# Attention and two gated layers on one core: the order of evictions and weight parts in the second step of a block, and a shorter start

## What is computed

```python
scores = 0.125 * q @ k.T                      # 2 batches x 8 heads, 768 positions, 64 wide
keep   = (key < n_global) | (0 <= query - key < n_local)      # 8 and 96
scores = where(keep, scores - slope[head] * dist, -1e9)
a      = exp(scores - max); a = a / (sum(a) + 1e-9)
x      = (a @ v) laid out as 1536 tokens x 512
h = x @ w_in;   g = h * sigmoid(h);           x = g @ w_out     # 512 -> 2048 -> 512
h = x @ w_in2;  g = h * clip(h + 3, 0, 6) / 6;  y = g @ w_out2
```

## Time and profile before

| what | value |
|---|---|
| runs | 586.82, 587.07, 587.07 us; median 587.07 |
| the profiled execution: its own time | 586.97 us |
| its span, first to last instruction | 585.2 us |
| PE busy | 580.0 us (99%) |
| DVE busy, ACT busy, POOL busy | 361.9, 335.5, 266.7 us |
| chain of work that ended last | PE 97% |

### The profile page before, as it was taken

How to read it: one execution, slowest core, us unless ns; L and a number is a source line. 1 busy time by engine, 2 the same in 40 slices (tenths; PEclk the granted TensorE clock), 3 DMA queues, 4 the chain that set the end, 5 groups by cost and what they waited for, 6 DMA issues and landing times.

```text
span 585.2 us, 9670 instructions
## 1 busy us (share of the span) xinstructions
PE 580.0 (99%) x3476; PEld 522.5 (89%) x3476; DVE 361.9 (62%) x669; ACT 335.5 (57%) x652; POOL 266.7 (46%) x282
## 2 busy tenths in 40 slices
PE   9999999999999999999999999999999999999998
PEld 6788899999999999999999989999988988889996
DVE  7777887657545775586556685475448765555331
ACT  7998976554444774444447575445546754455441
POOL 6678774678333044394333343593330443331110
DMA  6665500422222122212221222222211262211002
GB/s 238 256 237 191 204 7 2 144 72 73 73 73 72 36 73 73 73 43 101 73 72 37 73 72 73 74 72 73 71 46 30 70 216 72 71 37 38 1 0 108
DMA packets 14883, 50.05 MB, mean 86 GB/s; under 512 B 1650, under 2 KB 2162, under 8 KB 14834
## 3 DMA queue, kind: packets, MB, share of 16 engines
q1 hardware_dynamic: 14402, 48.63, 24.5%
q10 hardware_dynamic: 432, 0.79, 0.4%
HBM read 46.27 MB, written 3.15 MB: 84 GB/s over the span
## 4 chain that ended last, share of the span: by engine, by line
PE 97%; DVE 1%; ACT 1%; issue 0%; DMA 0%; DVEq 0%
PE ps L1152 40%; PE ps L1243 23%; PE ps L1234 15%; PE ps L1235 8%; PE ps L1100 3%; PE ps L1124 3%; PE ps L1076 3%; PE ps L1109 1%; ACT probs L842 1%; DVE negs L623 0%; DMA words<-in_counts 0%; ACT probsT L853 0%; DVEq L232 0%; DVE m_base L568 0%; DVE x_raw L641 0%
## 5 line engine op out<-in xcount | busy, mean ns | idle before, releaser
L404 POOL TENSOR_TENSOR wo_lo<-wo_raw,wo_hi 128x1024 fp32r<-128x1024 f32 x32 | 77.3, 2415 | 260.1 <-ACT wo_hi L907 257.0
L1152 PE MATMUL ps<-x_hi,wi_hi 128*128 128x384 f32 x448 | 150.8, 337 | 0.1
L1152 PE MATMUL ps<-x_hi,wi_lo 128*128 128x384 f32 x448 | 150.0, 335 | 0.0
L1152 PE MATMUL ps<-x_lo,wi_hi 128*128 128x384 f32 x448 | 150.0, 335 | 0.0
L599 DVE TENSOR_TENSOR c_sb<-ps,p_c 128x384 f32<-128x384 f32 x64 | 35.6, 557 | 161.7 <-PE ps L1152 161.5
L887 ACT ACTIVATE p_c<-ps 128x384 f32<-128x384 f32 x64 | 31.5, 492 | 127.4 <-PE ps L1152 127.1
L1152 PEld LDWEIGHTS ps<-x_hi,wi_hi 128*128 128x128 f32 x448 | 84.1, 188 | 3.4 <-ACT u_c L887 0.9
L1152 PEld LDWEIGHTS ps<-x_hi,wi_lo 128*128 128x128 f32 x448 | 84.1, 188 | 0.7
L1152 PEld LDWEIGHTS ps<-x_lo,wi_hi 128*128 128x128 f32 x448 | 84.1, 188 | 0.0
L1243 PE MATMUL ps<-wo_hi,g_lo 128*128 128x512 f32 (+1 forms) x194 | 76.3, 393 | 0.0
L1243 PE MATMUL ps<-wo_lo,g_hi 128*128 128x512 f32 (+1 forms) x194 | 76.3, 393 | 0.0
(11 more groups left out here) (113 smaller groups left out, 1064.3 us busy)
## 6 DMA issues: line engine op xcount, KB each, us to landing
wi_raw<-in_w_in SPq DMA_DIRECT2D x32, 512.0 KB, 3.4
wo_raw<-in_w_out SPq DMA_DIRECT2D x32, 512.0 KB, 3.4
v_raw<-in_v SPq DMA_DIRECT2D x8, 704.0 KB, 4.0
k_raw<-in_kT SPq DMA_DIRECT2D x7, 464.0 KB, 5.1
out_y<-y_out SPq DMA_DIRECT2D x11, 256.0 KB, 4.1
q_raw<-in_qT SPq DMA_DIRECT2D x6, 384.0 KB, 6.0
q_raw<-in_qT ACTq DMA_DIRECT2D x1, 384.0 KB, 4.6
k_raw<-in_kT SPq DMA_DIRECT2D x1, 320.0 KB, 3.7
```

The source lines that it names most:

```text
L404: nc.gpsimd.tensor_tensor(wo_lo[:, s % 2, :], wo_raw[:, s % 2, :], wo_hi[:, s % 2, :], ALU.subtract).then_inc(wo_lo_ok, 1)
L1152: mm = nc.tensor.matmul(p_bank(bank), w[:, s % 2, at], x[:, b, k, :], start=fresh and k == 0 and i == 0, stop=k == 1 and i == 2, skip_grou ...
```

## The change

Three edits. In the steps called evict: on ACT `wo_high(s)` moves from before keep(P6) to behind y_copy(4); on DVE y_copy(3) comes from the end of the step before to behind c_sum(0), and w_low(s+1, 1) goes from behind c_sum(0) to behind c_sum(2). At the start: two of the three operations that lead to flag no longer depend on each other, `rows` becomes a zeroed 128x128 piece of y_out, the matmul that spreads the numbers has 128 columns in place of 5, one idle matmul fewer stands ahead of it, and POOL waits for `own_ok` before its two-input operation on the band tile (it waited for it later). In the attention: copy_t(2) goes from ACT to DVE, behind negations(2).

```diff
-        rows = sb("rows", [P, 9])
-        cnt = rows[0:1, :]
+        tests = sb("tests", [1, 2])
...
+        ones, rows = y_out[:, 0, 0:P], y_out[:, 1, 0:P]
+        cnt = y_out[0:1, 1, 0:P]
...
         def copied(u):
-            return (pt_dve, u // 2) if u % 2 and u > 1 else (pt_act, u + 1 if u < 2 else u // 2 + 2)
+            if u in (0, 1):
+                return pt_act, u + 1
+            if u == 2:
+                return pt_dve, 1
+            return (pt_dve, u // 2 + 1) if u % 2 else (pt_act, u // 2 + 1)
...
                 pool.wait_ge(far_ok, 1)
+                pool.wait_ge(own_ok, 1)
                 nc.gpsimd.tensor_tensor(m_base[:, BAND], rel8[:, BAND], far[:, BAND], ALU.subtract).then_inc(band_link, 1)
...
-                pool.wait_ge(own_ok, 1)
                 for r in range(NR):
...
-            nc.vector.memset(y_out[:, 0, 0:P], 1.0).then_inc(idle_ok, 1)
-            nc.vector.memset(rows[:, 4:9], 0.0).then_inc(chain, 1)
+            nc.vector.memset(ones, 1.0).then_inc(idle_ok, 1)
+            nc.vector.memset(rows, 0.0).then_inc(chain, 1)
...
+            nc.vector.tensor_scalar(tests[:, 0:1], cnt[:, 5:6], -1.0, MAXLOC + 1.0, ALU.mult, ALU.add).then_inc(chain, 1)
+            nc.vector.tensor_scalar(tests[:, 1:2], cnt[:, 4:5], float(GLOB), -NEVER, ALU.is_gt, ALU.mult).then_inc(chain, 1)
+            links[0] += 2
...
-            link(nc.vector.tensor_scalar(cnt[:, 0:1], cnt[:, 5:6], 1.0, None, ALU.is_ge))
-            link(nc.vector.scalar_tensor_tensor(cnt[:, 0:1], cnt[:, 5:6], float(MAXLOC), cnt[:, 0:1], ALU.is_le, ALU.mult))
-            nc.vector.scalar_tensor_tensor(flag[:, :], cnt[:, 4:5], float(GLOB), cnt[:, 0:1], ALU.is_le,
-                                           ALU.mult).then_inc(flag_ok, 1)
+            dve.wait_ge(chain, links[0])
+            nc.vector.scalar_tensor_tensor(flag[:, :], tests[:, 0:1], cnt[:, 5:6], tests[:, 1:2], ALU.mult,
+                                           ALU.is_gt).then_inc(flag_ok, 1)
...
-                nc.vector.tensor_copy(nums[:, :], ps[:, 1, 0:5]).then_inc(nums_ok, 1)
+                nc.vector.tensor_copy(nums[:, :], ps[:, 1, 4:9]).then_inc(nums_ok, 1)
...
                 negations(2)
+                copy_t(2)
                 negations(3)
...
                 if evict:
-                    w_low(s + 1, 1)
+                    y_copy(blk - 1, 3)
                     y_copy(blk - 1, 5)
                 c_sum(s, 1, 0, p5_c, P7)
                 c_sum(s, 2, 1, u2_c, P3)
+                if evict:
+                    w_low(s + 1, 1)
...
                     if blk > 0 and f == 0:
                         y_copy(blk - 1, 1)
-                        y_copy(blk - 1, 3)
...
                 exps(4)
-                copy_t(2)
                 exps(5)
...
                 if evict:
                     w_high(s + 1, 1)
                     y_copy(blk - 1, 2)
-                wo_high(s)
+                else:
+                    wo_high(s)
                 keep(s, u2_c, 0, P6)
                 keep(s, p5_c, 1, P5)
                 if evict:
                     y_copy(blk - 1, 4)
+                    wo_high(s)
...
-            busy(4)
+            busy(3)
             pe.wait_ge(row_ok, 3)
-            nc.tensor.matmul(ps[:, 1, 0:5], y_out[:, 0, 0:P], rows[:, 4:9], start=True, stop=True).then_inc(rows_ok, 1)
+            nc.tensor.matmul(ps[:, 1, 0:P], ones, rows, start=True, stop=True).then_inc(rows_ok, 1)
             busy(2)
```

More of the change, by code:

```diff
@@ L1057, in busy @@
                 for _ in range(n):
-                    nc.tensor.matmul(ps[:, 0, 0:P], y_out[:, 0, 0:P], y_out[:, 0, 0:P], start=True, stop=True)
-            busy(4)
+                    nc.tensor.matmul(ps[:, 0, 0:P], ones, ones, start=True, stop=True)
+            busy(3)
             pe.wait_ge(row_ok, 3)
-            nc.tensor.matmul(ps[:, 1, 0:5], y_out[:, 0, 0:P], rows[:, 4:9], start=True, stop=True).then_inc(rows_ok, 1)
+            nc.tensor.matmul(ps[:, 1, 0:P], ones, rows, start=True, stop=True).then_inc(rows_ok, 1)
             busy(2)
```

## The result

The changed kernel takes 581.84 us (median of 6 runs, 581.80 to 582.01) against 586.90 for the kernel before beside it (6 runs, 586.82 to 587.07): a ratio of 0.9913, 95% interval 0.9901 to 0.9926. The forecast was 585.4. The sign was right, but 5.06 us were gained and 1.66 forecast.

A forecast was written before the change was run, and what follows sets the result against it. PE, busy 99% of the span, bounds the kernel, so only its late starts can gain. Second steps 1.23 plus start 0.43 gave 1.66 us off 586.97: 585.31, as median 585.4; own range 584.95 to 585.9, over the cases 584.9 to 586.5.

The forecast's parts named there:

- Second steps: Products of steps 9, 17 and 25: two late PE starts go, 7.69 to 7.28 us each, 1.23 us in all.
- Margins of 0.37: In step 9, ACT is free 0.37 us before keep(P6) is due, DVE 0.37 us before c_sum(0).
- Rival B: Second steps: another wait ends almost as late, so only 0.4 there, with the start 0.83, 586.25 us; chance 0.1.
- The moved work costs nothing: Second steps: delayed wo_high, wo_low and w_low fit beside PE's about 8 us of `down` before the next products; cost nothing.
- Rival D: Steps 10, 18, 26: w_low's delay makes DVE late for c_sum(0), costing PE from 230.4 on, 588.6 at 231.5; chance 0.05.
- The start: Before PE's x_scaled wait ends at 18.93: flag, own_ok and band tile 0.1, copy_t(2) 0.33; 0.43 us, between 0.1 and 0.55.
- Rival C: Start: a PE gap of about 0.15 before the number matmul makes the clock rise later, costing 1.5, 586.9 us; chance 0.06.
- four rivals: B, C and D have own lines; A: only second steps gain, the start's gain is taken back, 585.85 us, chance 0.14.
- the three signs named as making me wrong: P5 or P7 still late in second steps; late P5 in the steps after; PE records of 0.21 us beyond 8.
- the lower end of 584.95: Whole kernel: the lower bound of the forecast's own range, 584.95 to 585.9 us.

The follow-up runs named there:

- g at 192: The kernel before with g_hi and g_lo moved by 32 bytes, alone or with every other tensor behind rows: 589.35 or 589.31 us.
- g at 128: The kernel before with only g_hi and g_lo moved, by 224 bytes, to 128 modulo 256, no instruction changed: 583.38 us, ratio 0.9941.
- everything by 128: The changed kernel with 128 unused bytes ahead of all SBUF tensors, so all distances between them stay: 581.79 us, ratio 0.9914.
- PE's operands by 128: The changed kernel with x, wi, wo and g (high and low) moved by 128 bytes modulo 256, all other tensors left: 581.82 us, ratio 0.9915.

## Why the forecast was wrong

**Second steps: right.** Two late starts, together 0.41 us, three times, all gained: 1.23 in the trace, 1.21 alone. Margins of 0.37 were forecast; DVE and ACT showed waits of 0.24 and 0.26. Rival B (a second wait) didn't come.

**The moved work costs nothing: right, with its mechanism.** Step 9's products start at 211.69 after and at 212.38 before, so the forecast's instants are compared from there. w_low was to run only from the end of wo_low on. wo_low was forecast to end 8.7 us (221.1 - 212.38) behind that start and ended 8.60 behind it (217.89 + 2.40 - 211.69); w_low was forecast to end 9.7 behind it and ended 9.55 behind it (218.44 + 2.80 - 211.69), 2.80 us long in place of 1.08. This agrees with the Trainium skill, SBUF — State Buffer, § Who interferes with whom, which the prediction weighed. What that section says of holding the ports for a whole instruction, it says of VectorE's 2-port modes; that a two-input operation waits until the other has ended is what this trace shows. The gates took about 0.5 each, as forecast (three in 1.48), since POOL's sums started only at 225.09, behind them. The sums fell beside the two later w_low instead, which took 3.18 in place of 2.09: 1.1 lost, where 1.8 was allowed. DVE was through 16.8 us behind the products' start (at 228.48), not 17.5 (229.9 - 212.38), and waited 0.92 for the next c_sum(0), where the bounds left 0.2 and "more likely by a microsecond" was said. Rival D had its mechanism right, but from the products' start DVE stayed 1.2 us short of the 18.0 (230.4 - 212.38) from which it would cost.

**The start: right within its range.** Nums was forecast at 3.77 and came at 3.80; line 568's 0.24 was 0.26; line 430 from 5.12, 5.20; line 575 at 6.38, 6.40; turn_inverses(1) near 18.5, 18.42. In total 0.51 against 0.43, within 0.1 to 0.55; by the medians of the single parts, 0.37 + 0.07 = 0.44.

**Rival C: the clock rose earlier, but the edit isn't shown to be the reason.** Timeline of PE in the start, after:

```profile
5.30 1.13 PE L1091 MATMUL ps<-k_raw,q_raw 64*128 64x256 f32 x8
6.68 0.44 PE L1115 MATMUL ps<-ident,probs 128*128 128x128 f32 x2 [0.25 <-ACT probs L855]
7.62 1.14 PE L1091 MATMUL ps<-k_raw,q_raw 64*128 64x256 f32 x8 [0.51 <-DVE negmax L634]
```

The first eight records of 256 columns take 1.13 us, not 1.75, so here they run at the higher level. (The profile gives the granted clock as 1.00 from the first microsecond on in both kernels, so the level is read from the records.) The traces of kernels with the same instructions in the start differ just as much:

| instructions of the start | kernel | first eight records, us | turn_inverses(1) at |
|---|---|---|---|
| before | g at 192 | 1.13 | 18.82 |
| before | g at 128 | 1.27 | 18.80 |
| before | the kernel before | 1.75 | 18.93 |
| before | second steps' order alone | 1.85 | 19.03 |
| changed | the changed kernel | 1.13 | 18.42 |
| changed | everything by 128 | 1.69 | 18.43 |
| changed | PE's operands by 128 | 1.70 | 18.40 |

So the instant of the rise isn't set by the edit alone. In the changed start a late rise is absorbed in PE's waits of 0.25 and 0.51 for ACT and DVE; in the old start it reaches turn_inverses(1). About 0.1 us of the 0.51 (18.93 - 18.80) hangs on the late rise in the one trace of the kernel before; against traces of the old start with an earlier rise the gain is 0.38 to 0.40. That the total of 0.51 lies so near the upper end of the forecast is in part luck of that trace.

**The step that failed.** It is the sentence that ends the first part: "Behind that I found PE without a gap worth counting, so what the start gains is what this instant moves." There were no gaps, but the sum 1.23 + 0.43 = 1.66 also took PE's pace behind that instant as fixed: it put at nothing, without a reason, what the edit does to the duration of the matmuls it doesn't touch. That term measured 3.4 us (3.46 where g's place alone was changed). The prediction costed the new `rows` as a memset of 0.1 us in DVE's wait, and not as 32 bytes by which every later tensor moves. With the places put back the sum is right: 585.21 against 585.4. None of the four rivals held the case, and the three signs named as making me wrong all stayed away; the missing sign was the duration of the matmuls that the change didn't touch. Two slips in the working changed nothing: the lower end of 584.95 is below what the terms themselves reach (587.07 - 1.23 - 0.55 = 585.29), and rival C's 0.1 us more for each record is (1.75 - 1.14) / 8 = 0.08 by its own rows, 1.8 us for 24 and not 2.4.

**What stays open.** Which operands must stand alike is shown, but not why. That `down1` is slowed by the place of x and wi, which only the matmuls before and after it read, might come of something that is carried from one stretch of matmuls into the next. But the second layer's `down` stands between the same products and isn't slowed. The two differ in their roles: in the first layer wo is loaded as weights and g streams past it, in the second g is loaded and wo streams. No run tested either. Nor was x moved against wi, a high part against its low part, or g to a place below 128 (32, 64 or 96).

## What to carry to other kernels

When a kernel is bound by PE, compare the durations of matmuls that the edit doesn't touch before explaining a gain: a changed size of any tensor moves all tensors behind it, and here that was twice the effect of the edit itself. To price an edit alone, pad so that the operands' places stay. And try the pad as a change in its own right: here the best of the places tried had all of PE's operands alike modulo 256 bytes.

## What the runs showed of the hardware that I had not expected

The second layer's `down`, a back-to-back stream of matmuls with F32R operands, 512 columns wide, ran at a pitch of 228 ns (8.20 / 36) or 233 ns (8.40 / 36) for the same instructions, with the mean granted clock at 1.000 both times. Which of the two it was went with the places of g and wo against one another modulo 256 bytes in SBUF. The same in the kernel's time: 581.8 us with all four pairs alike, 584.7 with x and wi apart from wo and g, 585.2 to 587.6 with g apart from wo. In the kernel before, g at 128, 160 and 192 gave 583.4, 586.8 and 589.3 us.
